# The padded halves of the attention state, summed from PSUM instead of copied from the state in SBUF

## The chip, the cores and the metric

The program runs on one core of a Trainium2 chip (trn2). The time is the device time of one execution in microseconds (us). Three runs of the kernel before gave 302.97, 303.89 and 305.05 us; the median is 303.89. Lower is better.

The core has five engines with a queue each: TensorE multiplies (its weight loads, PEld in the rows, run beside its matmuls, PE), VectorE (DVE) and ScalarE (ACT) work on SBUF and PSUM, GpSimd (POOL) on SBUF, and SyncE (SP) issues most of the transfers. An engine runs its queue in the order in which it is written; engines wait for one another by semaphores. PSUM has eight banks, and SBUF is the large memory on the chip.

## What is computed

Three parts follow one another. The first is a gated linear attention (batch 2, 8 heads, 768 tokens, head size 40). Per head it keeps a state C (40 x 40) and a vector n (40):

```
m_new  = max(f + m, i);  f_stab = exp(f + m - m_new);  i_stab = exp(i - m_new)
C = f_stab * C + i_stab * outer(v, k)
n = f_stab * n + i_stab * k
y = sigmoid(o) * (C @ q) / max(|n . q|, 1)
```

The second is an MLP over tokens and then one over channels, each with a residual and with a relu between its two products (768 -> 256 -> 768, 320 -> 1536 -> 320). The third is a gated projection: sigmoid of a causal convolution of five taps over x, times x @ w_val, the product times w_out. All is float32.

## The kernel before

The attention is done by chunks of 128 tokens: six per batch, twelve in all, numbered u. Within a chunk it is a masked product of q and k, weighted by exponentials of gate sums; between chunks the state is carried. A step is `attention(b, n)` with u = 6b + n, and n runs from 0 to 6: step n makes the masked product of chunk n, updates the state with chunk n and finishes y of chunk n - 1. All engines have a function of this name, and its order of lines is the order of the engine's queue.

The large products elsewhere are made more exact by splitting each float32 factor into a rounded part and a remainder (`_hi`, `_lo`): ScalarE makes hi of a weight (L671), GpSimd mostly lo (L539, L543), and TensorE runs three products for one. These splits of the later parts' weights (tok, ch, val, out) are laid among the attention's steps, by tables at the head of the program (`HI_AT`, `LO_POOL_AT`, `LO_VECTOR_AT`). Their staging buffers are shared: the load of a piece (`LOAD_AT`, issued by ScalarE at L397) waits until the piece before it in the same buffer has been split.

The steps of the first batch stand alone. After each of them from n = 4 on comes one chunk's share of the token MLP (`token_hidden`, L1252), which needs y_hi and y_lo of that chunk. The steps of the second batch are laid among the channel MLP of the first quarter of the tokens (L1177, L1315).

The state lies in SBUF as `state`, 104 partitions x 164: heads 0 to 3 in partitions 0 to 63, heads 4 to 7 in 64 to 103. The product that reads it (L1196) takes 128 rows, and it must see one group of heads at a time. So `apart` holds two padded copies, group 0 in one and group 1 in the other, with zeros elsewhere; there are two buffers of it, used in turn by even and odd chunks.

In step n of either batch VectorE runs in this order (n from 1 to 4; outside these some parts are missing):

1. multiplies the exponentials by q.k from PSUM, twice (`prob`, L958);
2. sums the new state: `delta` in PSUM, made by TensorE, plus `kept`, the decayed old state in SBUF (L969; in step 0 a copy, L966). This releases delta's PSUM bank;
3. finishes y of the chunk before: `den` (L978), the remainder `y_lo` of the chunk before that one (L948), `den` (L982), `rden` (L985), `yt` (L988);
4. makes the exponents of the next chunk, eight instructions (L939). ScalarE turns them into exponentials in place (L700);
5. copies the two halves of `state` into `apart` (L1003) and signals `apart_ready`.

GpSimd's step: `kept` (L583) from state and decay, `qs` = q times decay (L593), half of a weight's remainder (L539), `y` = yt times the output gate (L605, L606), which waits for yt, and `wv` (L572) for the next chunk. In the last step of the first batch VectorE makes this y itself (L1010, L1011). The last `token_hidden` of the first batch follows; ScalarE's `y_hi` for it stands behind ScalarE's split of a weight piece (L671) in that step.

PSUM's two banks `shared` serve all the small products (delta, y, hidden units and others) in turn; TensorE starts a product in one only when its last content was read (`begin`, L1166). In the second batch a step's delta, y and the hidden units before and behind them (`h_hi` L831 by ScalarE, `h_lo` L1107 by VectorE) share them.

## Time and profile before

| | before |
|---|---|
| median of three runs | 303.89 us |
| profiled execution | 303.86 us |
| its span, first to last instruction | 302.0 us |
| busy: TensorE matmul / weight load | 270.7 / 258.9 us |
| busy: VectorE | 203.2 us |
| busy: ScalarE / GpSimd | 122.6 / 88.0 us |
| transfers | 25.70 MB |

The profiled execution is 1.9 us longer than its span; what lies outside is start and end. In the page's 40 slices of 7.55 us each TensorE's matmuls are at 0.9 or more from 68 us on, up to the last three slices, and at 0.5 to 0.9 in most slices before. A busy time says how long an engine had an instruction under way: one that was under way but held up counts as busy.

### The profile page before, as it was taken

The page shows a single profiled execution, that of the slowest core. Times are in us where ns is not written, and L with a number is a line of the kernel's source. Part 1 is how long each engine was busy: PE and PEld are TensorE (multiplying, and loading weights), DVE is VectorE, ACT ScalarE, POOL GpSimd, SP SyncE. Part 2 cuts the span into 40 slices and gives each one's busy share as a digit, 9 for nine tenths or more (in the row PEclk, how much of TensorE's full clock was granted, in tenths as well). Part 3 has the DMA queues.
Part 4 walks back from the last instruction along what each step waited for, and adds up shares of the span by engine and source line. Part 5 has one row for each costly group of instructions (what it writes and reads, how often), then busy time and mean ns, then how long its engine had stood idle before and what let it go on. Part 6 is the DMA issues. An engine that isn't in the chain of part 4 may idle for free.

```text
span 302.0 us, 5376 instructions
## 1 busy us (share of the span) xinstructions
PE 270.7 (90%) x2024; PEld 258.9 (86%) x2024; DVE 203.2 (67%) x415; ACT 122.6 (41%) x225; POOL 88.0 (29%) x102
## 2 busy tenths in 40 slices
PE   0689678759999999999999999999999999999875
PEld 0577567659989999999899999999999999999774
DVE  7989999785698667866776521534674048762693
ACT  2656465226945453254333222432223333222623
POOL 4435755650066554324500400000012000040440
PEclk9959979796999999999999999999999999999979
DMA  7599964515567235322000001000000100000011
GB/s 219 159 305 306 294 178 123 174 30 208 173 161 243 77 90 150 88 80 67 0 0 3 0 22 46 0 2 0 0 3 0 64 4 0 2 0 1 24 43 65
DMA packets 26289, 25.70 MB, mean 85 GB/s; under 512 B 13976, under 2 KB 22008, under 8 KB 26264
## 3 DMA queue, kind: packets, MB, share of 16 engines
q1 hardware_dynamic: 21976, 18.72, 21.2%
q10 hardware_dynamic: 4288, 6.64, 6.8%
q8 instruction: 16, 0.26, 0.4%
q14 instruction: 9, 0.07, 0.1%
HBM read 23.34 MB, written 2.02 MB: 84 GB/s over the span
## 4 chain that ended last, share of the span: by engine, by line
PE 62%; DVE 10%; ACT 4%; issue 3%; DMA 2%; POOL 2%; ACTq 0%; DVEq 0%; POOLq 0%
PE shared L1177 25%; PE h_ps L1315 18%; DVE prob L939 3%; PE shared L1280 2%; PE s_ps L1215 2%; PE s_ps L1252 2%; PE shared L1265 2%; PE hv_ps L1196 2%; PE hv_ps L1200 1%; DMA stage<-val 1%; PE s_ps L1436 1%; DVE y_lo L948 1%; PE h_ps L1252 1%; PE shared L1284 1%; POOL x L628 1%
## 5 line engine op out<-in xcount | busy, mean ns | idle before, releaser
L1107 DVE SCALAR_TENSOR_TENSOR h_lo<-shared,h_hi 128x384 fp32r<-128x384 f32 x48 | 26.4, 557 | 35.0 <-ACT h_hi L831 34.8
L1315 PE MATMUL h_ps<-ch_hi,h_hi 128*128 128x320 f32 x144 | 45.4, 315 | 0.0
L831 ACT ACTIVATE h_hi<-shared 128x384 fp32r<-128x384 f32 x48 | 23.2, 489 | 53.5 <-PE shared L1177 50.7
L1315 PE MATMUL h_ps<-ch_hi,h_lo 128*128 128x320 f32 x144 | 44.5, 309 | 0.0
L1315 PE MATMUL h_ps<-ch_lo,h_hi 128*128 128x320 f32 x144 | 44.3, 308 | 0.0
L1177 PE MATMUL shared<-u_hi,ch_hi 128*128 128x384 f32 x96 | 32.9, 342 | 0.6 <-DVE yt L988 0.3
L1177 PE MATMUL shared<-u_lo,ch_hi 128*128 128x384 f32 x96 | 32.5, 339 | 0.0
L1177 PE MATMUL shared<-u_hi,ch_lo 128*128 128x384 f32 x96 | 32.5, 339 | 0.0
L1215 PE MATMUL s_ps<-q_in,k_in 128*128 128x128 f32 x192 | 27.5, 303 | 3.6 <-DMA q_in<-qT 3.5
L1215 PEld LDWEIGHTS s_ps<-q_in,k_in 128*128 128x128 f32 x192 | 25.6, 214 | 5.5 <-DMA q_in<-qT 4.2
L1043 DVE SCALAR_TENSOR_TENSOR gate<-x,conv_sb,gate 128x384 f32<-128x384 f32 x44 | 29.0, 667 | 1.0
L1315 PEld LDWEIGHTS h_ps<-ch_hi,h_hi 128*128 128x128 f32 x144 | 27.1, 188 | 0.4 <-DVE yt L988 0.2
L700 ACT ACTIVATE prob<-prob 128x512 f32<-128x512 f32 x24 | 14.9, 630 | 30.0 <-DVE prob L939 30.0
L1315 PEld LDWEIGHTS h_ps<-ch_lo,h_hi 128*128 128x128 f32 x144 | 27.1, 188 | 0.0
L1315 PEld LDWEIGHTS h_ps<-ch_hi,h_lo 128*128 128x128 f32 x144 | 27.0, 188 | 0.0
L1196 PE MATMUL hv_ps<-qs,apart 128*41 128x128 f32 x160 | 17.4, 298 | 7.0 <-DVE prob L958 6.4
L1200 PE MATMUL hv_ps<-prob,v_in 128*41 128x128 f32 x192 | 20.2, 304 | 1.2 <-DVE prob L958 1.2
L958 DVE TENSOR_TENSOR prob<-s_ps,prob 128x512 f32<-128x512 f32 x24 | 15.9, 687 | 7.7 <-PE s_ps L1215 7.5
L539 POOL TENSOR_TENSOR ch_lo<-stage,ch_hi 128x640 fp32r<-128x640 f32 (+1 forms) x8 | 13.3, 1680 | 21.7 <-ACT ch_hi L671 21.7
L1177 PEld LDWEIGHTS shared<-u_hi,ch_hi 128*128 128x128 f32 x96 | 18.0, 188 | 1.4 <-DVE yt L988 0.7
L605 POOL TENSOR_TENSOR y<-yt,o_sig 128x320 f32<-128x320 f32 x11 | 11.2, 1020 | 24.3 <-DVE yt L988 24.3
L1177 PEld LDWEIGHTS shared<-u_hi,ch_lo 128*128 128x128 f32 x96 | 18.0, 188 | 0.0
(191 smaller groups left out, 636.6 us busy)
## 6 DMA issues: line engine op xcount, KB each, us to landing
G_all<-G_scratch SPq DMA_DIRECT2D x11, 512.0 KB, 5.0
o_sig<-on ACTq DMA_DIRECT2D x2, 960.0 KB, 6.0
k_in<-kT SPq DMA_DIRECT2D x24, 80.0 KB
q_in<-qT SPq DMA_DIRECT2D x24, 80.0 KB
kn_in<-kn SPq DMA_DIRECT2D x12, 160.0 KB, 4.3
v_in<-vn SPq DMA_DIRECT2D x12, 160.0 KB, 4.8
stage<-ch ACTq DMA_DIRECT2D x3, 640.0 KB, 4.3
out<-o_sb SPq DMA_DIRECT2D x12, 160.0 KB, 1.8
```

The source lines that it names most:

```text
L539: eng.tensor_tensor(lo[:, half], raw[:, half], hi[:, half].bitcast(F32), ALU.subtract).then_inc(split[p], 1)
L605: pool.tensor_tensor(y32[:, 0:DM], yt[:], og, ALU.mult)
L700: act.activation(prob[w % 4][:], prob[w % 4][:], ACT.Exp).then_inc(exp_ready, 1)
L831: act.activation(h_hi[i % 3][:], ps_of(key)[:, 0:T], ACT.Relu).then_inc(hi_ready, 1)
L958: dve.tensor_tensor(prob[w % 4][:], s_ps[g][:], prob[w % 4][:], ALU.mult).then_inc(prob_ready, 1)
L1043: return dve.scalar_tensor_tensor(out=gate[:, d, :], in0=xt, scalar=w, in1=gate[:, d, :], op0=ALU.mult, op1=ALU.add)
L1107: took(dve.scalar_tensor_tensor(out=h_lo[i % 3][:], in0=ps_of(key)[:, 0:T], scalar=0.0, in1=h_hi[i % 3][:].bitcast(F32), op0=ALU.max, op1= ...
L1177: last = pe.matmul(out_ap, w, x, start=(n == 0), stop=(n == len(terms) - 1))
L1196: pe.matmul(hv_ps[64 * g:64 * g + D1, tile_cols(j)], apart[v % 2][:, g, j * D1:(j + 1) * D1], qs[v % 2][:, tile_cols(j)], start=True, stop ...
L1200: last = pe.matmul(hv_ps[64 * g:64 * g + D1, tile_cols(j)], v_in[v % 3][:, g * HG + j, :], prob[(2 * v + g) % 4][:, tile_cols(j)], start=( ...
L1215: last = pe.matmul(s_ps[g][:, tile_cols(j)], k_in[k_buffer(u)][:, g, tile_cols(j)], q_in[k][:, tile_cols(j)], start=True, stop=True)
L1315: last = pe.matmul(h2_ps[t][:, 0:DM], a[:, tile_cols(t)], w[:, f, :], start=(f == 0 and n == 0), stop=(f == FT - 1 and n == 2))
```

## The change

The two halves of `apart` are no longer copied from `state` at the step's end. They are summed (in step 0 copied) straight from delta's PSUM bank and `kept`, where the state is summed, each over its own partitions, and ahead of the state itself. `state` is still needed for the next `kept`, so its sum stays, but not in step 4, after which the batch needs no further state; there VectorE waits for its own last sum and releases the bank by an increment. The waits that guarded the copies move along: for the hidden matmuls that read this buffer of `apart` (`hv_ready`), and, at the start, for the zeroing of both buffers.

```diff
--- before.py
+++ after.py
@@ -959,14 +959,27 @@
                 if n < NC - 1:
                     key = ("delta", u)
                     full(dve, key)
-                    if u > 0:
-                        dve.wait_ge(apart_ready, with_next(u - 1))
-                    new, ps = state[:], ps_of(key)[0:ROWS, 0:HG * D1]
-                    if n == 0:
-                        took(dve.tensor_copy(new, ps), key)
+                    if u >= 1:
+                        dve.wait_ge(hv_ready, u)
+                    if n >= 1:
+                        dve.wait_ge(kept_ready, with_both(u))
+
+                    def grown(dst, r):
+
+                        ps = ps_of(key)[r, 0:HG * D1]
+                        if n == 0:
+                            return dve.tensor_copy(dst, ps)
+                        return dve.tensor_tensor(dst, ps, kept[r, :], ALU.add)
+
+                    new = apart[(u + 1) % 2]
+                    grown(new[0:64, 0, :], slice(0, 64))
+                    last = grown(new[64:ROWS, 1, :], slice(64, ROWS)).then_inc(apart_ready, 1)
+                    if n < NC - 2:
+                        last = grown(state[:], slice(0, ROWS))
+                        took(last, key)
                     else:
-                        dve.wait_ge(kept_ready, with_both(u))
-                        took(dve.tensor_tensor(new, ps, kept[:], ALU.add), key)
+                        dve.wait_ge(apart_ready, with_next(u))
+                        dve.sem_inc(shared_done[J[key] % 2], 1)
                 if (b, n) in LO_VECTOR_AT:
                     make_lo(dve, *LO_VECTOR_AT[b, n])
                 if n >= 1:
@@ -992,16 +1005,8 @@
                         ALU.mult), y_key)
                 if u == 0:
                     columns(1)
-                    dve.wait_ge(apart_zeroed, 2)
                 if n + 1 < NC:
                     exponents(u + 1)
-                if n < NC - 1:
-                    if u >= 1:
-                        dve.wait_ge(hv_ready, u)
-                    done(dve, key)
-                    for g, r in enumerate((slice(0, 64), slice(64, ROWS))):
-                        last = dve.tensor_copy(apart[(u + 1) % 2][r, g, :], state[r, :])
-                    last.then_inc(apart_ready, 1)
                 if (b, n) == (0, NC):
 
                     dve.wait_ge(o_ready, b + 1)
@@ -1073,6 +1078,7 @@
                     last.then_inc(a_lo_ready, 1)
 
             exponents(0)
+            dve.wait_ge(apart_zeroed, 2)
             for n in range(ATT_STEPS):
                 attention(0, n)
             exponents(NC, (0,))
```

VectorE's queue, first batch, from the end of step 3 (exponents of chunk 4) into step 4. `prob_`, `apart_` are buffers with their numbers; in brackets stands what an instruction waits for. Before:

```order
L939 SCALAR_TENSOR_TENSOR prob_109<-G_all_106,A_col,h_ps 128x128 x3
L1003 COPY apart_117<-state 64x164 [waits shared_done1,hv_ready]
L1003 COPY apart_117<-state 40x164
L958 TENSOR_TENSOR prob_108<-s_ps,prob_108 128x512 [waits s_ready,exp_ready]
L958 TENSOR_TENSOR prob_109<-s_ps,prob_109 128x512 [waits s_ready,exp_ready]
L969 TENSOR_TENSOR state<-shared,kept 104x164 [waits kept_ready,apart_ready,shared_full]
L978 TENSOR_SCALAR den<-shared 128x8 [waits shared_full]
L948 TENSOR_TENSOR y_lo<-y_121,y_hi 128x384 [waits split0,y_hi_ready]
L982 SCALAR_TENSOR_TENSOR den<-shared,den 128x8 [waits vector_step]
```

Now:

```order
L939 SCALAR_TENSOR_TENSOR prob_109<-G_all_106,A_col,h_ps 128x128 x3
L958 TENSOR_TENSOR prob_108<-s_ps,prob_108 128x512 [waits s_ready,exp_ready]
L958 TENSOR_TENSOR prob_109<-s_ps,prob_109 128x512 [waits s_ready,exp_ready]
L972 TENSOR_TENSOR apart_118<-shared,kept 64x164 [waits kept_ready,hv_ready,shared_full]
L972 TENSOR_TENSOR apart_118<-shared,kept 40x164
L991 TENSOR_SCALAR den<-shared 128x8 [waits apart_ready,shared_full]
L948 TENSOR_TENSOR y_lo<-y_121,y_hi 128x384 [waits split0,y_hi_ready]
L995 SCALAR_TENSOR_TENSOR den<-shared,den 128x8 [waits vector_step]
```

The copies between the exponents and the multiplications are gone; two sums follow the multiplications. This is step 4, in which the state's own sum is left out.

VectorE's queue, second batch, step 0, between the last multiplication and the hidden units `h_lo` of the channel MLP. Before:

```order
L966 COPY state<-shared 104x164 [waits apart_ready,shared_full]
L939 SCALAR_TENSOR_TENSOR prob_110<-G_all_107,A_col,mask_sb 128x128 [waits G_in1,hv_ready]
L939 SCALAR_TENSOR_TENSOR prob_110<-G_all_107,A_col,mask_sb 128x128 x3
L939 SCALAR_TENSOR_TENSOR prob_111<-G_all_107,A_col,mask_sb 128x128 [waits G_in1]
L939 SCALAR_TENSOR_TENSOR prob_111<-G_all_107,A_col,mask_sb 128x128 x3
L1003 COPY apart_118<-state 64x164 [waits shared_done0,hv_ready]
L1003 COPY apart_118<-state 40x164
L1107 SCALAR_TENSOR_TENSOR h_lo_87<-shared,h_hi_84 128x384 [waits hi_ready]
```

Now:

```order
L971 COPY apart_118<-shared 64x164 [waits hv_ready,shared_full]
L971 COPY apart_118<-shared 40x164
L971 COPY state<-shared 104x164
L939 SCALAR_TENSOR_TENSOR prob_110<-G_all_107,A_col,mask_sb 128x128 [waits G_in1,hv_ready]
L939 SCALAR_TENSOR_TENSOR prob_110<-G_all_107,A_col,mask_sb 128x128 x3
L939 SCALAR_TENSOR_TENSOR prob_111<-G_all_107,A_col,mask_sb 128x128 [waits G_in1]
L939 SCALAR_TENSOR_TENSOR prob_111<-G_all_107,A_col,mask_sb 128x128 x3
L1113 SCALAR_TENSOR_TENSOR h_lo_87<-shared,h_hi_84 128x384 [waits hi_ready]
```

The halves moved from behind the eight exponent instructions to a place ahead of them; they are copies from PSUM here, and the state's copy follows them.

## Rows read from the trace of the kernel before

**Rows 1.** Busy time by stretch, core 0.

```profile
15.00:67.00 52.00, 38.73 (x396) 34.69 (x396) 47.66 (x105) 25.12 (x39) 29.67 (x30) 0.86 0.69 201
67.00:82.00 15.00, 14.93 (x78) 14.19 (x79) 10.26 (x24) 11.29 (x16) 0.00 (x0) 0.79 0.55 180
82.00:140.00 58.00, 57.41 (x555) 53.84 (x554) 42.80 (x104) 26.09 (x47) 28.54 (x30) 1.00 0.45 131
```

**Rows 2.** The chain that ended last, first batch: start us, us, what.

```profile
52.48 0.73 DVE apart L1003
```

**Rows 3.** The removed copies in the second batch: ns min/median/max.

```profile
L1003 DVE COPY apart<-state x10: 226/238/244, 89.1 to 129.2; 64x164 f32<-64x164 f32 x5, 40x164 f32<-40x164 f32 x5
```

**Rows 4.** All copies together; then VectorE in time, steps 2 to 4.

```profile
L1003 DVE COPY apart<-state 64x164 f32<-64x164 f32 (+1 forms) x20 | 15.1, 757 | 0.1
...
34.37 3.97 DVE L1003 COPY apart<-state 64x164 f32<-64x164 f32 x2
...
43.25 3.72 DVE L1003 COPY apart<-state 64x164 f32<-64x164 f32 x2
...
51.89 2.36 DVE L1003 COPY apart<-state 64x164 f32<-64x164 f32 x2
```

**Rows 5.** GpSimd in time: start us, us, line, operation, idle before it.

```profile
29.33 1.80 POOL L539 TENSOR_TENSOR tok_lo<-stage,tok_hi 128x768 fp32r<-128x768 f32 x1
...
34.09 0.74 POOL L572 TENSOR_TENSOR wv<-v_in,w_col 128x328 f32<-128x328 f32 x1 [0.47 <-DMA v_in<-vn]
...
36.43 1.80 POOL L539 TENSOR_TENSOR tok_lo<-stage,tok_hi 128x768 fp32r<-128x768 f32 x1
41.35 0.87 POOL L605 TENSOR_TENSOR y<-yt,o_sig 128x320 f32<-128x320 f32 x1 [3.12 <-DVE yt L988]
...
44.80 1.82 POOL L539 TENSOR_TENSOR tok_lo<-stage,tok_hi 128x768 fp32r<-128x768 f32 x1
49.99 0.87 POOL L605 TENSOR_TENSOR y<-yt,o_sig 128x320 f32<-128x320 f32 x1 [3.37 <-DVE yt L988]
...
52.33 1.82 POOL L539 TENSOR_TENSOR tok_lo<-stage,tok_hi 128x768 fp32r<-128x768 f32 x1
...
61.94 3.85 POOL L539 TENSOR_TENSOR ch_lo<-stage,ch_hi 128x768 fp32r<-128x768 f32 x2 [1.62 <-ACT ch_hi L671]
```

**Rows 6.** VectorE instructions that read PSUM, by line and in time.

```profile
L969 DVE TENSOR_TENSOR state<-shared,kept x8: 319/319/330, 23.3 to 123.2; 104x164 f32<-104x164 f32 x8
...
L958 DVE TENSOR_TENSOR prob<-s_ps,prob x24: 680/691/693, 15.6 to 133.2; 128x512 f32<-128x512 f32 x24
...
29.05 0.32 DVE L969 TENSOR_TENSOR state<-shared,kept 104x164 f32<-104x164 f32 x1
```

**Rows 7.** Second batch, step 1: VectorE, TensorE, and TensorE's wait for h_lo.

```profile
92.36 0.32 DVE L969 TENSOR_TENSOR state<-shared,kept 104x164 f32<-104x164 f32 x1
...
93.28 0.34 PE L1177 MATMUL shared<-u_hi,ch_hi 128*128 128x384 f32 x1
...
PE shared L1226 <- DVE h_lo L1107: 0.6, 1, 0.6
```

**Rows 8.** VectorE instructions with two SBUF operands, first batch, in time.

```profile
29.35 2.20 DVE L948 TENSOR_TENSOR y_lo<-y,y_hi 128x384 fp32r<-128x384 f32 x1
...
39.88 0.55 DVE L948 TENSOR_TENSOR y_lo<-y,y_hi 128x384 fp32r<-128x384 f32 x1
...
62.26 1.87 DVE L1010 TENSOR_TENSOR y<-yt,o_sig 128x320 f32<-128x320 f32 x1
64.05 1.82 DVE L1011 TENSOR_TENSOR y<-yt,o_sig 128x64 f32<-128x64 f32 x1
```

**Rows 9.** The weight transfer (KB, us to landing) and ScalarE behind it.

```profile
stage<-ch ACTq DMA_DIRECT2D x1, 768.0 KB, 6.1
...
60.31 1.49 ACT L671 ACTIVATE ch_hi<-stage 128x1536 fp32r<-128x1536 f32 x1
```

**Rows 10.** TensorE's restart after the first batch, in time.

```profile
67.07 0.63 PE L1252 MATMUL h_ps<-y_hi,tok_hi 128*128 128x320 f32 x1 [3.40 <-DVE y_lo L948]
```

## The prediction

> **What bounds the kernel now.** I read the stretches first [rows 1]; the columns are the stretch, its length, the busy time of TensorE's matmuls, of its weight loads, of VectorE, ScalarE and GpSimd, then granted clock, DMA share and GB/s. While the second batch's attention runs between other matmuls (82 to 140 us) TensorE is busy 57.41 of 58.00 us, so only what makes it wait counts. In the first batch's attention (15 to 67 us) TensorE has 38.73 of 52.00 us and VectorE 47.66: this stretch is VectorE's. The chain of waits agrees: the second copy of step 4 stands in it [rows 2]. I call the step with index n "step n".
>
> Next, the 20 copies that the change removes. In the second batch the ten take 226 to 244 ns each, one after another [rows 3]. All 20 take 15.1 us, so the first batch's five pairs take 12.7, against 0.48 us a pair unhindered; those of steps 2, 3 and 4 take 3.97, 3.72 and 2.36 us [rows 4]. GpSimd explains it [rows 5]: in step 2 its wv starts at 34.09 and its queue runs without a gap to the end of tok_lo at 38.23; the copies start at 34.37 and end at 38.34. A copy from SBUF to SBUF waits for GpSimd here, and, with that queue back to back, for several of its instructions in a row.
>
> By the Trainium skill ("SBUF — State Buffer", Who interferes with whom) a float32 copy within SBUF may run in a two-port mode and then needs the port pair that GpSimd uses, while a VectorE instruction with at most one SBUF input outside these modes does not contend. Both halves agree with this trace: 3.97 us beside a busy GpSimd, and the next rows.
>
> What replaces the copies reads PSUM and at most one SBUF operand. All eight state sums take 319 to 330 ns and all 24 multiplications by s_ps 680 to 693 [rows 6]; the sum at 29.05 ran while GpSimd was about to pass from qs to tok_lo (29.33) and was not stretched. So I price a half at 0.32 us, not stretched.
>
> **The change part by part.**
> Two copies less per step, five steps per batch. First batch: on VectorE's path, and 12.7 us is the ceiling. Second batch: nothing comes back. The copies stood behind the eight exponent instructions, and what waits on those (the exponentials on ScalarE, then h_hi, then h_lo) had been released already.
>
> Two sums (or PSUM copies in step 0) more per step, now ahead of y and of the exponents. From the rows one sum takes 0.32 us whole; the next instruction behind the state sum at 92.36 overlapped its end, so two cost between 0.48 (the time of a copy pair) and 0.64 us [rows 3, 6]. I take the upper end, since no row shows halves overlapping. The skill ("VectorE: DVE Perf Modes", Two Vector instructions with no wait between them) says that an instruction whose output starts in another quadrant than the last one waits until that has finished; this speaks against the change. By it the ten steps would pay 6.4 us, without it 4.8.
>
> In step 4 of each batch the state sum goes (0.32 less), and a wait of VectorE for its own sums and an increment come in. No row prices it; between nothing and 0.32 us, a whole sum's time, it cancels at worst what goes.
>
> The buffer's bank is released after three reads, 0.64 us later. The tightest place is step 1 of the second batch: the state sum ran 92.36 to 92.68, and TensorE's next product started at 93.28 [rows 7]; 0.60 us of slack against 0.64. The wait for the hidden matmuls costs nothing: the same step's delta product stands behind them in TensorE's queue. The wait for the zeroed buffers, moved to the start, is long over.
>
> **What is late next.** Removing a stall only pays up to the next one, so I walk the first batch.
> Steps 0 and 1: the exponents of step 1 and what follows move by under 0.5 us either way; then y_lo at 29.35 took 2.20 us and ended at 31.55, 0.42 after GpSimd's tok_lo (29.33 to 31.13) [rows 5, 8]. y_lo has two SBUF operands and is held as the copies are. It ends then whether it comes early or not: no gain up to here, 34.37.
> Step 2: the exponents end at 34.37, and step 3 can begin. From the end of the copies (38.34) to y_lo (39.88) were 1.54 us; with 0.64 more y_lo is asked for at 36.6, or a microsecond later behind an exponential. GpSimd's tok_lo runs until 38.23, so y_lo ends at 38.65 where it ended at 40.43 (its 0.55 us began at 39.88) [rows 8]. Gain 1.78, not 3.97.
> From there GpSimd sets the pace: yt releases GpSimd's y, then come wv, kept, qs, tok_lo, then y_lo, den, rden, yt. From the start of y at 41.35 to the end of tok_lo at 46.62 are 5.27 us [rows 5]; 0.42 for y_lo's end and, from there to the next y, the 0.92 between 40.43 and 41.35 make 6.6, against 8.64 (y at 41.35 and 49.99). Gain 2.0 more. So y of step 4 starts near 46.2 in place of 49.99; from it to the end of tok_lo, 54.15, are 4.16 us as before, and that end comes near 50.4, 3.75 earlier.
> That tok_lo frees the buffer for the next weight transfer. It took 6.1 us and ScalarE's ch_hi started right behind it, at 60.31 [rows 9]. Now 50.4 + 6.1 = 56.5, ch_hi to 58.05, y_hi to 58.55. The last y_lo meets the first half of GpSimd's ch_lo (3.85 us for two, 1.9 each, from 58.05), ends at about 60.3, and TensorE starts the last token_hidden. It started at 67.07 [rows 10]. Gain 6.7: 3.75 from the transfer, 2.95 because VectorE's two y products, 1.87 and 1.82 us beside ch_lo at 62 to 66 [rows 8], now run before ch_lo does.
> If y_lo waits for both halves of ch_lo, 1.9 us go: gain 4.8. If the transfer is faster by a microsecond, gain 7.7.
> Behind 67 the chain is TensorE, ScalarE and loads in the same order, and moves with it.
>
> Second batch: in step 0 the 0.64 us stand ahead of the exponents, whose exponentials hold up h_hi and h_lo, and TensorE waited 0.6 us for h_lo already [rows 7]. I charge 0.6 here and nothing elsewhere, between 0 (the exponents were held by GpSimd's ch_lo anyway) and 1.0.
>
> **The sum.** 303.86 (profiled execution; the median of three is 303.89) - 6.7 + 0.6 = 297.8. The forecast's own range is a gain of 4.8 - 1.0 to 7.7 + 0.3: 295.8 to 300.1.
>
> **Rivals.**
> 1. *The loads pace it.* If the weight transfer at 50.4 lands 3 us later, since everything ahead of it on the queues is now packed closer, ch_hi and the last y_lo are 3 us later: gain 3.7 - 0.6, 300.8. For it: DMA share 0.69 in the stretch [rows 1], and 6.1 us for the transfer. Against: the transfer of G ahead of it moves by about as much. Chance 0.13.
> 2. *More than computed.* TensorE pauses for less before the last token_hidden than the 3.40 us of [rows 10], and keeps its clock. From 67 to 82 us it was granted 0.79 of it [rows 1]; with only the two levels of 2.4 and 1.2 GHz that is 6.3 us of 15 at the lower one, and at the upper these would take 3.1 less. Two thirds of it: 295.7. Against: ScalarE and the loads share this path. Chance 0.08.
> 3. *Slower: the second batch pays and the first gives nothing.* Place: the shared bank at [rows 7], in every step with 0.6 us of slack or less. Price 0.64 us in five steps, 3.2 in all; with y_lo and tok_lo taking the whole of the first batch's stall, 307.1. It decides if the sums halt TensorE in each step; most have more slack, and 3.97 and 3.72 us of stall have nothing to fill them. Chance 0.05.
> 4. *No change.* The halves read from PSUM are held by GpSimd as the copies were, because kept lies in SBUF: then VectorE stands as before, 303.9 to 304.9. 32 unstretched instructions speak against [rows 6], though few of the state sums lay beside a busy GpSimd. Chance 0.09.
> The forecast keeps 0.65.
>
> **Numbers.** A change of 1% (3.0 us) is about what can be told here. Faster by more (below 300.9): forecast, rival 2 and most of rival 1, 0.84. Within: 0.11. Slower: 0.05. Forecast and rival 1 hold 0.78, so the range goes from 295.3, into rival 2, to 300.9.
>
> **What would show it.** The half sums at 0.32 us beside a busy GpSimd; y_lo in steps 3, 4 and 5 stretched to 1.3 us and more and ending 0.4 us after tok_lo; GpSimd's y of step 4 near 46.2; the last token_hidden near 60.3; the two y products near 0.4 us. In the second batch about 1.2 us of waiting for h_lo in place of 0.6. It is wrong if the half sums are stretched, if TensorE restarts within 2 us of 67, or if its waits after 82 grow beyond 1.5 us.

## The result, and the profile after

Four runs of the changed kernel gave 298.65, 299.74, 300.29 and 300.83 us, median 300.01; four of the kernel before gave a median of 304.39. The ratio is 0.985 with a 95% interval of 0.982 to 0.989: 1.5% faster. The ratios in this document leave out runs that took over 1.5% longer than the fastest of their kernel, two of four in experiment 5 and two of ten in experiment 7. The forecast was 297.8 (295.3 to 300.9), faster with 0.84. The profiled execution took 298.65 us with a span of 296.9, against 303.86 and 302.0: 5.1 us less in the spans; it is the fastest of the four.

These are the stretches of the changed kernel, with the columns of [rows 1]; the cuts lie where the same work begins, 7 to 8 us earlier than there.

```profile
15.00:60.00 45.00, 36.42 (x412) 32.72 (x411) 38.84 (x106) 25.53 (x39) 27.81 (x30) 0.92 0.83 244
60.00:75.00 15.00, 14.72 (x86) 13.72 (x87) 10.37 (x25) 12.05 (x17) 2.09 (x2) 0.89 0.53 175
75.00:144.00 69.00, 65.83 (x602) 61.22 (x600) 54.57 (x116) 28.37 (x54) 34.67 (x37) 1.00 0.37 105
```

The first batch is 7 us shorter and VectorE's busy time in it falls from 47.66 to 38.84. The third line is the second batch up to the first `x` that follows it; the same stretch before the change is

```profile
83.00:149.00 66.00, 65.08 (x600) 61.08 (x599) 48.80 (x117) 28.95 (x54) 34.66 (x37) 1.00 0.38 110
```

So the first batch gave more than was forecast, and the second took some of it back: 3 us more for the same work, with TensorE idle for 3.17 us of it where it was idle for 0.92.

VectorE's groups by line answer [rows 4, 6]: busy us and mean ns of one. L972 and L971 are the new half sums and half copies (20 in all, 16 + 4), L939 with mask_sb the exponents of the second batch, L1015 and L1016 the last y products of [rows 8].

```profile
L939 DVE SCALAR_TENSOR_TENSOR prob<-G_all,A_col,mask_sb 128x128 f32<-128x128 f32 x40 | 21.4, 603 | 0.0
L948 DVE TENSOR_TENSOR y_lo<-y,y_hi 128x384 fp32r<-128x384 f32 x12 | 15.1, 1261 | 2.4 <-ACT y_hi L707 2.2
L972 DVE TENSOR_TENSOR apart<-shared,kept 64x164 f32<-64x164 f32 (+1 forms) x16 | 5.2, 322 | 0.1
L971 DVE COPY apart<-shared 64x164 f32<-64x164 f32 (+1 forms) x4 | 1.3, 320 | 0.0
L1015 DVE TENSOR_TENSOR y<-yt,o_sig 128x320 f32<-128x320 f32 x1 | 0.5, 493 | 0.1
L1016 DVE TENSOR_TENSOR y<-yt,o_sig 128x64 f32<-128x64 f32 x1 | 0.2, 219 | 0.0
```

15.1 us of copies became 6.5 us of half sums. The exponents were 17.3 us before (mean 500 ns) and `y_lo` 11.1 (925 ns): what the copies no longer wait for, two other kinds of instruction wait for in part.

VectorE and then GpSimd in time, from steps 3 to 5 of the first batch, and the last `y_lo` (compare [rows 4, 5, 8]):

```profile
36.17 0.66 DVE L972 TENSOR_TENSOR apart<-shared,kept 64x164 f32<-64x164 f32 x2
37.17 1.74 DVE L948 TENSOR_TENSOR y_lo<-y,y_hi 128x384 fp32r<-128x384 f32 x1
...
44.12 1.40 DVE L948 TENSOR_TENSOR y_lo<-y,y_hi 128x384 fp32r<-128x384 f32 x1
...
58.17 1.92 DVE L948 TENSOR_TENSOR y_lo<-y,y_hi 128x384 fp32r<-128x384 f32 x1 [0.91 <-ACT y_hi L707]
```

```profile
36.67 1.82 POOL L539 TENSOR_TENSOR tok_lo<-stage,tok_hi 128x768 fp32r<-128x768 f32 x1
39.83 0.87 POOL L605 TENSOR_TENSOR y<-yt,o_sig 128x320 f32<-128x320 f32 x1 [1.34 <-DVE yt L1001]
...
46.44 0.86 POOL L605 TENSOR_TENSOR y<-yt,o_sig 128x320 f32<-128x320 f32 x1 [1.33 <-DVE yt L1001]
...
48.77 1.81 POOL L539 TENSOR_TENSOR tok_lo<-stage,tok_hi 128x768 fp32r<-128x768 f32 x1
```

The half sums at 36.17 lie within GpSimd's `qs` and the start of `tok_lo` (its queue is busy from 34.32 to 38.49) and still take 0.33 us each; `y_lo` behind them is held and ends at 38.91, 0.42 after `tok_lo`. The last `tok_lo` ends at 50.58, the weight transfer issued at 50.61 lands after 5.6 us, and ScalarE and TensorE follow (answering [rows 9] and [rows 10]):

```profile
56.24 1.49 ACT L671 ACTIVATE ch_hi<-stage 128x1536 fp32r<-128x1536 f32 x1 [1.17 <-DMA stage<-ch]
```

```profile
60.15 0.41 PE L1258 MATMUL h_ps<-y_hi,tok_hi 128*128 128x320 f32 x1 [2.66 <-DVE y_lo L948]
```

The second batch, step 2, in time: VectorE, then GpSimd.

```profile
94.36 0.67 DVE L972 TENSOR_TENSOR apart<-shared,kept 64x164 f32<-64x164 f32 x2
95.06 0.33 DVE L972 TENSOR_TENSOR state<-shared,kept 104x164 f32<-104x164 f32 x1
95.37 1.91 DVE L948 TENSOR_TENSOR y_lo<-y,y_hi 128x384 fp32r<-128x384 f32 x1
98.04 6.28 DVE L939 SCALAR_TENSOR_TENSOR prob<-G_all,A_col,mask_sb 128x128 f32<-128x128 f32 x8
```

```profile
95.29 1.58 POOL L539 TENSOR_TENSOR ch_lo<-stage,ch_hi 128x640 fp32r<-128x640 f32 x1 [3.20 <-ACT ch_hi L671]
98.20 0.92 POOL L605 TENSOR_TENSOR y<-yt,o_sig 128x320 f32<-128x320 f32 x1 [1.33 <-DVE yt L1001]
...
100.18 0.80 POOL L572 TENSOR_TENSOR wv<-v_in,w_col 128x328 f32<-128x328 f32 x1 [0.74 <-DMA v_in<-vn]
100.94 0.51 POOL L583 TENSOR_TENSOR kept<-state,decay 104x164 f32<-104x164 f32 x1
101.41 1.26 POOL L593 TENSOR_TENSOR qs<-q_in,decay 128x512 f32<-128x512 f32 x1
102.64 1.53 POOL L539 TENSOR_TENSOR ch_lo<-stage,ch_hi 128x640 fp32r<-128x640 f32 x1
```

Before, the same step read, on VectorE and on GpSimd:

```profile
102.77 0.55 DVE L948 TENSOR_TENSOR y_lo<-y,y_hi 128x384 fp32r<-128x384 f32 x1
...
104.07 3.36 DVE L939 SCALAR_TENSOR_TENSOR prob<-G_all,A_col,mask_sb 128x128 f32<-128x128 f32 x8
```

```profile
103.11 1.63 POOL L539 TENSOR_TENSOR ch_lo<-stage,ch_hi 128x640 fp32r<-128x640 f32 x1 [3.10 <-ACT ch_hi L671]
...
107.78 0.74 POOL L572 TENSOR_TENSOR wv<-v_in,w_col 128x328 f32<-128x328 f32 x1 [1.82 <-DMA v_in<-vn]
```

`y_lo` used to start 0.34 us ahead of `ch_lo`; now it starts 0.08 behind it and takes 1.36 us more. The exponents therefore start late, and GpSimd's next chain (`wv`, `kept`, `qs`, `ch_lo`), which used to start after their end, now runs through them: 6.28 us in place of 3.36, ending with that chain. TensorE's waits after 74 us show what it costs (us in total, times, longest), where there were 0.6 for `h_lo` [rows 7] and 0.3 for `yt`, and the row in time shows the longer of the two at the `delta` product of the step behind:

```profile
PE shared L1232 <- DVE h_lo L1113: 2.3, 2, 1.9
PE shared L1183 <- DVE yt L1001: 0.9, 1, 0.9
```

```profile
106.01 0.76 PE L1232 MATMUL shared<-wv,kn_in 128*64 128x41 f32 x16 [1.85 <-DVE h_lo L1113]
```

### The profile page after: what moved, and what is told of

Same layout as the page of the kernel before. It is cut to its first block, busy times and chain, and to the rows that moved or that the text cites. A ratio compares the mean times of both kernels' runs of the same rounds, so it can differ in the third digit from the quotient of the medians.

```text
span 296.9 us, 5367 instructions
## 1 busy us (share of the span) xinstructions
PE 265.7 (90%) x2024; PEld 253.4 (85%) x2024; DVE 199.4 (67%) x413; ACT 121.7 (41%) x225; POOL 88.0 (30%) x102
## 4 chain that ended last, share of the span: by engine, by line
PE 53%; DVE 22%; ACT 7%; issue 4%; DMA 4%; POOL 3%; ACTq 0%; DVEq 0%; POOLq 0%
PE shared L1183 24%; PE h_ps L1321 16%; DVE prob L939 9%; DVE y_lo L948 4%; DVE gate L1048 2%; PE s_ps L1221 2%; DMA stage<-ch 2%; PE shared L1286 2%; PE s_ps L1258 2%; DVE apart L972 1%; ACT prob L700 1%; PE shared L1271 1%; DVE prob L958 1%; DMA stage<-val 1%; POOL x L628 1%
## 5 line engine op out<-in xcount | busy, mean ns | idle before, releaser
L939 DVE SCALAR_TENSOR_TENSOR prob<-G_all,A_col,mask_sb 128x128 f32<-128x128 f32 x40 | 21.4, 603 | 0.0
L1206 PE MATMUL hv_ps<-prob,v_in 128*41 128x128 f32 x192 | 18.7, 285 | 1.4 <-DVE prob L958 1.4
```

The lines of the kernel that those rows point to most:

```text
L939: last = dve.scalar_tensor_tensor(out=prob[(2 * u + g) % 4][:, tile_cols(j)], in0=G_all[u % 2][:, tile_cols(h)], scalar=A_col[:, col:col + ...
L1206: last = pe.matmul(hv_ps[64 * g:64 * g + D1, tile_cols(j)], v_in[v % 3][:, g * HG + j, :], prob[(2 * v + g) % 4][:, tile_cols(j)], start=( ...
```

## The experiments

Two theories stood at the start. **A**: the first batch gains as walked, and the second loses because VectorE comes later there and its instructions with two SBUF inputs now overlap GpSimd's. **B** and **C** in the expectations are the rivals each of them names. In what follows two lengths are read from each profile: from the start to the first `h_lo` of the channel MLP (the first batch and what hangs on it), and from there to the first `x` behind the second batch. What comes after is the same in all 13 profiles: 152.9 to 153.1 us to the end of the span. With them goes what happens in step 2 of the second batch:

```
                               first  h_lo    y_lo starts, us       wv starts behind   exponents
kernel                         h_lo   to x    (ch_lo starts)        the exponents      take
before                         83.03  65.96   102.77 0.55 (103.11)  3.71               3.36
changed                        74.96  68.96    95.37 1.91  (95.29)  2.14               6.28
changed, once more             75.73  69.14    96.12 1.90  (96.04)  1.87               6.28
first batch only               75.57  66.82    96.32 0.55  (96.66)  3.28               3.36
first batch only, once more    76.78  66.10    96.73 0.55  (97.08)  4.80               3.36
second batch only              83.78  66.65   104.19 0.55 (104.15)  3.84               3.34
place alone, both batches      77.46  69.58    98.31 1.77  (98.09)  1.93               6.28
place alone, first batch       77.32  65.86    97.06 0.55  (97.40)  4.24               3.36
source alone, first batch      75.94  65.94    95.65 0.55  (95.99)  3.37               3.36
first batch, delay in second   74.51  68.24    95.08 0.55  (95.02)  2.09               6.78
first batch, tok_lo behind y   79.80  65.84    99.52 0.55  (99.87)  4.53               3.35
changed, ch2_lo later          74.46  66.56    94.83 0.55  (none)   3.09               2.87
first batch, ch2_lo later      74.86  65.89    94.59 0.55  (none)   3.28               2.87
```

**1. The change in the first batch only.**

```diff
+                    if b == 0:
+                        ... (the sums of the halves, as in the change)
+                    else:
+                        ... (the state's sum, as before)
...
+                if n < NC - 1 and not (b == 0):
+                    ... (the copies behind the exponents, as before)
...
```

> The change in the first batch's steps alone; the second batch copies the halves from state behind the exponents as before. Theory A: in the changed kernel the first batch gained some 8 us by the time the second batch's attention begins, and 3 us were lost in the second batch, because the two sums ahead of y move VectorE's instructions with two SBUF operands (y_lo, exponents) 0.65 us later, into GpSimd's ch_lo, kept and qs. Then this kernel is about 3 us faster than the changed one, near 297 us; the 40 exponents of the second batch are back near 17 us (21.4 in the changed kernel) and TensorE's waits between the start of the second batch's attention and the third part stay below 1.5 us (3.5 in the changed kernel). Theory B: the loss comes from the first batch's being earlier, which shifts loads and ScalarE's ch_hi against GpSimd and VectorE; then the time stays near 300 and the exponents near 21 us.

Measured: median 296.38 us (295.17 to 299.35, six runs) against 304.15, ratio 0.974 (0.969 to 0.979): faster than the changed kernel. The exponents take 18.0 us, and TensorE restarts at

```profile
59.65 0.64 PE L1275 MATMUL h_ps<-y_hi,tok_hi 128*128 128x320 f32 x1 [3.54 <-DVE y_lo L948]
```

and never waits for `h_lo`. The whole gain is the first batch's. The weight transfer behind the last `tok_lo` takes 4.5 us here, and `ch_hi` starts at 53.71, 2.5 us ahead of the changed kernel's; TensorE's restart comes only 0.5 us sooner. GpSimd's `ch_lo`, from 55.34 on, now catches the second y product, and the last `y_lo` starts late:

```profile
55.67 1.83 DVE L1033 TENSOR_TENSOR y<-yt,o_sig 128x64 f32<-128x64 f32 x1
58.09 1.50 DVE L948 TENSOR_TENSOR y_lo<-y,y_hi 128x384 fp32r<-128x384 f32 x1 [0.59 <-ACT y_hi L707]
```

**2. The change in the second batch only.** The same edit with `b == 1`.

> The change in the second batch's steps alone. Theory A: nothing is won and the second batch loses, by 0.6 us where no new meeting with GpSimd comes about and by up to 3 where it does: 305 to 307.4 us. Theory B: as before, 304.4, within 0.5.

Measured: 306.16 us (303.76 to 307.63, ten runs), ratio 1.005 (1.001 to 1.010). The first batch's ten copies take 15.4 us (12.7 before). The profile shows 0.69 us more than before in the second stretch, but no stretched exponents: `wv` comes 3.84 us behind their start, too late to meet them.

```profile
104.19 0.55 DVE L948 TENSOR_TENSOR y_lo<-y,y_hi 128x384 fp32r<-128x384 f32 x1
...
105.49 3.34 DVE L939 SCALAR_TENSOR_TENSOR prob<-G_all,A_col,mask_sb 128x128 f32<-128x128 f32 x8
```

So in this profile moving the sums ahead costs 0.7 us by itself. The other 2.3 of the changed kernel need the meeting in step 2, and this kernel misses the first part of it by little: its `y_lo` starts 0.04 us behind `ch_lo` and isn't held. The profiled run (305.18) is among the shorter of the ten; the median lies 2.0 us above that of the kernel before, and what the longer runs met was not profiled.

**3. The place alone.** The halves are copied from `state` in SBUF as before, but right behind its sum, in both batches.

```diff
                         took(dve.tensor_tensor(new, ps, kept[:], ALU.add), key)
+                    if u >= 1:
+                        dve.wait_ge(hv_ready, u)
+                    done(dve, key)
+                    for g, r in enumerate((slice(0, 64), slice(64, ROWS))):
+                        last = dve.tensor_copy(apart[(u + 1) % 2][r, g, :], state[r, :])
+                    last.then_inc(apart_ready, 1)
... (the same lines behind the exponents go)
```

> The halves are still copied from state in SBUF, but right behind the state's sum, where the changed kernel sums them from PSUM (VectorE waits for its own sum first). It tells place from source. Theory A1 (source: only what reads PSUM escapes GpSimd): the copies are held by GpSimd in the first batch at the new place as well, and the time stays near 304. Theory A2 (place): at the new place the copies are held by qs and tok_lo, but y_lo right behind them was to be held until the end of the same tok_lo anyway, so the copies cost only some 0.3 us each, and the first batch gains nearly as much as in the changed kernel: 300 to 302 us, with the copies' busy time still well above 10 us.

Measured: 299.24 us (297.51 to 301.76), ratio 0.983 (0.977 to 0.990), as good as the changed kernel though the copies still read SBUF. VectorE in time, first batch, steps 3 and 4:

```profile
36.59 1.91 DVE L974 COPY apart<-state 64x164 f32<-64x164 f32 x2
38.72 0.56 DVE L948 TENSOR_TENSOR y_lo<-y,y_hi 128x384 fp32r<-128x384 f32 x1
43.91 1.91 DVE L974 COPY apart<-state 64x164 f32<-64x164 f32 x2
46.05 0.56 DVE L948 TENSOR_TENSOR y_lo<-y,y_hi 128x384 fp32r<-128x384 f32 x1
```

The copies are held to the end of the same `tok_lo` that would have held `y_lo`, which then runs free: one hold in place of the other. In the second batch this kernel meets GpSimd as the changed one does.

**4. The source alone.** First batch: the halves are summed from PSUM, but at the old place, behind the exponents, the bank released there. Second batch as before.

```diff
... (in the first batch the state's sum no longer releases the bank)
+                    if b == 0:
+                        half = ps_of(key)
+                        for g, r in enumerate((slice(0, 64), slice(64, ROWS))):
+                            dst, src = apart[(u + 1) % 2][r, g, :], half[r, 0:HG * D1]
...
+                                last = dve.tensor_tensor(dst, src, kept[r, :], ALU.add)
+                        last.then_inc(apart_ready, 1)
+                        dve.wait_ge(apart_ready, with_next(u))
+                        dve.sem_inc(shared_done[J[key] % 2], 1)
...
```

> The other half of the pair: in the first batch the halves are summed from PSUM and kept, but at the old place behind the exponents (the bank is released there); the second batch is as before. If the source alone is enough, the ten instructions take 0.32 us each and none is held, the first batch gains about 7 us until TensorE's restart, and the time is 296.5 to 298. If the place is what pays, 304. A later release of delta's bank could cost up to 1 us, since TensorE's next delta product waits for it.

Measured: 297.50 us (296.57 to 298.80), ratio 0.977 (0.972 to 0.983); the sums take

```profile
L1011 DVE TENSOR_TENSOR apart<-shared,kept 64x164 f32<-64x164 f32 (+1 forms) x8 | 2.6, 322 | 0.1
```

and TensorE restarts at 60.91. In the first batch the source alone brings most of the gain: 6.7 us of the medians, where experiment 1 beside it has 7.8, and the intervals of the two overlap. Experiment 10 tries the place alone there.

**5. The changed kernel once more.** No edit.

> The changed kernel as it is, beside the next three on one chip, and a second profile of it. If the second batch's loss comes from a meeting of VectorE's y_lo and exponents with GpSimd's queue, the second profile shows exponents stretched by microseconds at one or two of its steps again (sum of the 40 at 20 us or more, 17.3 before) and the time is 299 to 301 us.

Measured: median 299.45 us of four runs (295.07 to 299.91). Three of them lie at 299.2 to 299.9, and the ratio (0.976, 0.967 to 0.984) says little. The profile, of the run of 299.74, repeats the pattern:

```profile
96.12 1.90 DVE L948 TENSOR_TENSOR y_lo<-y,y_hi 128x384 fp32r<-128x384 f32 x1
98.78 6.28 DVE L939 SCALAR_TENSOR_TENSOR prob<-G_all,A_col,mask_sb 128x128 f32<-128x128 f32 x8
```

TensorE restarts as early as in the first profile of this kernel (60.15):

```profile
60.07 0.64 PE L1258 MATMUL h_ps<-y_hi,tok_hi 128*128 128x320 f32 x1 [2.74 <-DVE y_lo L948]
```

One run of 295.07 us stands apart. No profile of such a run exists; that in it `y_lo` was not held, as in experiment 2, is possible and not shown.

**6. The changed kernel, with GpSimd's remainder of the third piece of ch2 one step later.**

```diff
-              (1, 0): (6, 0), (1, 1): (6, 1), (1, 2): (7, 0), (1, 3): (7, 1),
+              (1, 0): (6, 0), (1, 1): (6, 1), (1, 3): (7, 0), (1, 4): (7, 1),
```

> The changed kernel, with GpSimd's splits of the last third of ch2 moved from steps 2 and 3 of the second batch to steps 3 and 4. Theory A (y_lo of step 2 met the ch_lo that starts as it does, so the exponents behind it met wv, kept, qs and the next ch_lo): y_lo of step 2 takes 0.55 us and not 1.9, the exponents of step 2 about 3 us and not 6.3, and up to 3 us come back, 297 to 298.5. Against it: the moved ch_lo meets the exponents or y_lo one step later, or TensorE waits for the third piece; then 299.5 or more.

Measured: 296.98 us (295.90 to 297.50), ratio 0.975 (0.971 to 0.978). VectorE, step 2, and the group of exponents:

```profile
94.83 0.55 DVE L948 TENSOR_TENSOR y_lo<-y,y_hi 128x384 fp32r<-128x384 f32 x1
96.14 2.87 DVE L939 SCALAR_TENSOR_TENSOR prob<-G_all,A_col,mask_sb 128x128 f32<-128x128 f32 x8
```

```profile
L939 DVE SCALAR_TENSOR_TENSOR prob<-G_all,A_col,mask_sb 128x128 f32<-128x128 f32 x40 | 16.0, 468 | 0.0
```

With `ch_lo` gone from step 2 the stretch falls from 68.96 to 66.56 us: 2.4 of the 3.0 us come back, and 0.6 stays, the price of the sums' place. This bears out theory A for the second batch.

**7. First batch only, with GpSimd's remainder of tok behind its y.** If `y_lo` waits for `tok_lo`, let it come first.

```diff
-                if (b, n) in LO_POOL_AT:
+                if b == 1 and (b, n) in LO_POOL_AT:
                     make_lo(pool, *LO_POOL_AT[b, n])
...
                                        ALU.mult).then_inc(y32_ready, 1)
+                if b == 0 and (b, n) in LO_POOL_AT:
+                    make_lo(pool, *LO_POOL_AT[b, n])
```

> As the kernel with the change in the first batch alone, and in the first batch GpSimd's weight split stands behind its y, not ahead of it. It asks whether y_lo held by tok_lo is what paces the first batch now. If so, y_lo takes 0.55 us in steps 2 to 4, but GpSimd's own round (y, split, wv, kept, qs) is as long as it was, 5.3 us plus 1.3, so each step is shortened by at most 0.5 us and the time is 295.5 to 297.5. If wv, kept and qs, which now stand behind the split, come late for TensorE, up to 2 us slower.

Measured: 303.42 us (ten runs, 300.55 to 307.00), ratio 0.997 (0.993 to 1.001): the gain is gone and the expectation missed. `y_lo` is free in steps 2 to 5 (0.55 to 0.63 us), but the split ends later, and the split is what others wait for:

```profile
PE h_ps L1277 <- POOL tok_lo L539: 2.5, 1, 2.5
```

```profile
55.91 1.80 POOL L539 TENSOR_TENSOR tok_lo<-stage,tok_hi 128x768 fp32r<-128x768 f32 x1
...
63.42 3.92 POOL L539 TENSOR_TENSOR ch_lo<-stage,ch_hi 128x768 fp32r<-128x768 f32 x2 [5.02 <-ACT ch_hi L673]
```

The last `tok_lo` ends at 57.71, where the two profiles of experiment 1's kernel have 49.20 and 50.39; the transfer starts behind it, and TensorE restarts at 65.70 in place of 59.65 and 60.86. That the end of the last `tok_lo` paces the end of the first batch is what the prediction rested on; here it is shown by delaying it. Whether the delay came by the transfer or by TensorE's own wait for `tok_lo` (the first row), this run doesn't separate.

**8. First batch only, with the delay of the second put in.** In the second batch half sums are made ahead of the state's sum and the copies stay, so VectorE is later by the sums and nothing else changes.

```diff
...
+                        for g, r in enumerate((slice(0, 64), slice(64, ROWS))):
+                            dst, src = apart[(u + 1) % 2][r, g, :], ps_of(key)[r, 0:HG * D1]
...
+                                dve.tensor_tensor(dst, src, kept[r, :], ALU.add)
...
```

> The kernel with the change in the first batch alone, and in the second batch the two half sums from PSUM are made as well, ahead of the state's sum, while the copies behind the exponents stay (the halves are written twice). Theory A: the 0.65 us ahead of y and the exponents is all that costs, so 3 us are lost again, near 299.5 us, with the exponents at 20 us or more. Theory C: the loss came with taking the copies away from behind the exponents (they kept VectorE off GpSimd's queue or the other way round); then it stays near 296.5.

Measured: 297.69 us (296.90 to 298.17), ratio 0.977 (0.974 to 0.980). The delay alone stretches the exponents to 21.9 us and makes TensorE wait 1.8 us for `h_lo`; the stretch is 68.24 us, 1.4 to 2.1 above the two profiles of the first batch only. The median is 1.3 us above that of experiment 1, which ran on another chip, and the intervals of the two ratios overlap; near 299.5 was expected. So it is the profile, and not the median, that shows the loss. Here `y_lo` started 0.06 us behind `ch_lo` and was not held; in the changed kernel it started 0.08 behind and was held; the exponents were caught all the same, since `wv`, which waits for `v_in`, started early, 2.09 us behind their start.

**9. The best of both.** First batch only, with the edit of experiment 6.

> The change in the first batch alone, as in the first experiment, and with it GpSimd's two halves of the remainder of the third piece of the second channel weight (ch2_lo) a step later (in steps 3 and 4 of the second batch, where they were in steps 2 and 3). Theory A (the first batch gives its 8 us whatever the second does; the second costs by what GpSimd and VectorE do at the same time in its step 2): nothing is stretched there any more, the 40 exponents take 16 to 17 us in all (18.0 in the first experiment, 21.4 in the changed kernel), TensorE starts the last token_hidden at 59.5 to 60.5, and the time is 295.5 to 296.5 us, 0.5 to 1 below the first experiment beside it. Rival (the exponents of the first experiment's second batch are held but behind nothing that TensorE waits for): the exponents are as short, and the time is that of the first experiment within 0.3 us. Rival B (what the faster first batch gives is lost again to the loads of the second batch): no gain, and waits for stage or weights in the stretch behind 75 us.

Measured: 296.44 us (295.48 to 298.20, six runs), ratio 0.975 (0.971 to 0.978). The exponents take 16.7 us and the second stretch 65.89, as before the change; but experiment 11 beside it has the same median. Once the exponents aren't caught, what is left of their stretching is hidden: the rival holds.

**10. The place alone, first batch only.** The edit of experiment 3 under `if b == 0`, the second batch as before.

> First batch alone again, but only the place is changed: the halves are still copied from state in SBUF, right behind the state's sum, ahead of y. The second batch is as before the change. Theory A2 (in the first batch the place suffices: the copies are held by GpSimd until tok_lo ends, but y_lo behind them would have been held by the same tok_lo, so one hold takes the place of the other): copies of steps 2 to 4 of about 1.9 us a pair, y_lo behind them 0.56 us, last token_hidden between 59.7 and 61.5, time 296.3 to 298.3, at most 1.5 us above the first experiment beside it. Rival (source alone: without the sums from PSUM the stall only moves): last token_hidden not before 64 and time above 300.

Measured: 298.25 us (295.82 to 299.52, six runs), ratio 0.980 (0.976 to 0.984), 1.8 us above experiment 11 where at most 1.5 was expected; TensorE restarts at 62.38, outside the expected 59.7 to 61.5. So the place alone brings some three quarters of the gain (6.1 us of the medians against 7.9). The rest is this:

```profile
37.31 1.91 DVE L975 COPY apart<-state 64x164 f32<-64x164 f32 x2
39.46 0.56 DVE L948 TENSOR_TENSOR y_lo<-y,y_hi 128x384 fp32r<-128x384 f32 x1
```

`y_lo` ends at 40.02, 1.14 us behind `tok_lo` (37.06 to 38.88), where in the changed kernel it ends 0.42 behind; GpSimd's period from one `tok_lo` to the next is 7.33 us (37.06 to 44.39) against 6.61 (36.67 to 43.28). With PSUM as source, what follows the sums already waits inside the hold.

**11. Experiment 1 once more, beside 9 and 10.** No edit.

> The first experiment (the change in the first batch alone) once more, beside the two others, so that they have something to be compared with on the same chip. Expected 296.4 us as before, between 295.5 and 297.5, a ratio to the kernel before of 0.970 to 0.980; last token_hidden at 59.5 to 60; exponents 18 us in all. If it is above 298 the spread between chips is as large as what the other two are to tell apart, and they decide nothing.

Measured: 296.45 us (294.39 to 298.57, six runs), ratio 0.974 (0.969 to 0.979), within 0.1 us of experiment 1. Its profiled run restarts at 60.86, a microsecond later than expected.

## Why the prediction was right, and where it was off

- **The copies waited for GpSimd, and the half sums don't**: 0.31 to 0.33 us each as priced (0.32), 20 of 20. A pair takes 0.65 to 0.67 us, the upper of the two ends. The rule of the Trainium skill that speaks against the change ("VectorE: DVE Perf Modes", Two Vector instructions with no wait between them) fits: the second half starts in another quadrant of partitions and doesn't overlap the first. The sum of 6.4 us by it compares with 6.5 measured.
- **y_lo is late next**: in steps 3 and 4 of the first batch it ended at 38.91 (38.65 forecast) and 45.52, each 0.42 to 0.43 behind `tok_lo`. GpSimd's period was 6.61 us against 6.6 forecast (39.83 to 46.44), y of step 4 came at 46.44 (46.2). In step 5 it took 0.61 us, where the prediction had wanted 1.3 or more: it started only 0.19 us ahead of the end of `tok_lo`, and ended 0.42 behind it; nothing hung on that.
- **The transfer and the restart**: `tok_lo` ended at 50.58 (50.4), `ch_hi` started at 56.24 (56.5), the y products took 0.49 and 0.22 us (about 0.4 wanted), TensorE restarted at 60.15 (60.3). The gain there is 6.92 us against 6.7. Experiment 7 shows that the end of `tok_lo` carries it. The branch "If the transfer is faster by a microsecond, gain 7.7" is wrong: in the two profiles of the first batch only it took 4.5 and 4.7 us, yet TensorE restarted 10.45 and 10.47 us behind the end of `tok_lo`, later than the changed kernel's 9.57. An earlier `ch_lo` catches the second y product (1.83 and 1.84 us in place of 0.22), and the last `y_lo` then ends 0.4 us behind the second half of `ch_lo`, not the first.
- **Rival 2, more than computed**, came true in part: from the restart to the first `h_lo` passed 14.81 us where it had been 15.96 (67.07 to 83.03), with 0.88 of the clock granted in that stretch against 0.80. TensorE had paused 2.66 us before its restart in place of 3.40. That gave 1.15 us in this run. The other profile of the changed kernel (experiment 5) paused 2.74 us and yet took 15.66, at a clock of 0.82: there it gave 0.30. Over all 13 profiles the stretch follows the granted clock, which at 1.00 is the upper of its two levels (2.4 GHz) throughout and below that a mix with the lower (1.2 GHz): 15.8 to 16.0 us at 0.80 and 0.81, 15.4 at 0.85, 14.8 to 15.1 at 0.88 and 0.89, 14.1 at 1.00 (experiment 7). The pause alone doesn't tell which it will be: 2.79 us in experiment 8 went with 0.89, 2.74 in experiment 5 with 0.82, and 3.54 with 0.81 in experiment 1 and 0.85 in experiment 3.
- **The second batch: the term that was mis-sized.** The step said: "I charge 0.6 here and nothing elsewhere, between 0 (the exponents were held by GpSimd's ch_lo anyway) and 1.0." It measured 3.0 us (68.96 against 65.96), 3.2 in the second profile. The 0.6 is there (0.69 in experiment 2, 0.60 in experiment 6, both without the meeting); the other 2.4 is a meeting with GpSimd in step 2, which no step of the prediction looked for. The hold of `y_lo` there starts the exponents 1.35 us late (11.79 us behind those of step 1, 10.44 before), and their stretching starts those of step 3 later by 1.26 more (11.79 against 10.53). The prediction walked the first batch instruction by instruction against GpSimd and charged the second by one wait. The text also named its own alarm, waits after 82 beyond 1.5 us: TensorE's waits for `h_lo` and `yt` are 3.2 where they were 0.9. By that sign the account of the second batch was wrong, though the total fell within the range.
- **Rivals 1, 3 and 4** did not come: the transfer took 5.6 us, not 9; the first batch gave all it had; the sums weren't held.

The sum then is 303.86 - 6.9 - 1.15 + 3.0 = 298.8, and the profiled execution took 298.65. Without the meeting it would have been 2.4 less (an estimate from experiment 6).

**Luck** is in it too. The forecast gain was 6.1 us, and the medians moved by 4.4; 300.01 lies 2.2 above the forecast and 0.9 inside the upper bound. That bound was set for a late transfer (rival 1), which did not come; the second batch used up the room. In the profiled run the clock gave back 1.15 us of that loss, in the other profile 0.30.

**Faster than both** is the change in the first batch only: 296.4 us in twelve runs on two chips, 3 to 3.6 below the changed kernel's medians, with a ratio (0.974, at most 0.979) clear of the changed kernel's 0.982 to 0.989. The changed kernel with `ch_lo` a step later (experiment 6, 297.0) comes close to it.

## What to carry to other kernels

Two engines that exclude each other on SBUF make a stall wherever their instructions meet, so an instruction moved by 0.6 us is priced by what it will run beside: write down, for the steps behind it too, which instruction of the other engine starts first. Apply such a change only where its stall is, since elsewhere it can bring only the delay. And of two engines that wait for one another, ask whose end others wait for before giving the other one the lead.

## What the runs showed of the hardware

- Who is held turns on less than 0.1 us. In step 2 of the second batch `y_lo` started 0.08 us behind `ch_lo` and took 1.9 us (in both profiles of the changed kernel); started 0.04 and 0.06 behind it (experiments 2 and 8), it took 0.55, and `ch_lo` took 2.01 and 2.04 in place of 1.58. GpSimd's times in a profile are rough, so the boundary itself isn't measured. The Trainium skill ("SBUF — State Buffer", Who interferes with whom) says that the port pair shared by VectorE and GpSimd is an exclusive lock, and that the order of issue decides which of the two is blocked; both outcomes occur here.
- The exponents (two SBUF inputs and a scalar per partition) are caught by chains: in step 2 of the second batch eight took 2.87 us free, 6.28 to 6.78 where GpSimd's `wv` started 1.87 to 2.14 us behind their start, and 3.36 or less where it started 3.09 or more behind. In step 3, in the kernels that had this meeting, `wv` started 1.4 us behind their start, no `ch_lo` stood behind `qs`, and they took 4.8. In step 2 `wv` starts when `v_in` has landed, which varied by 2.1 us against the first `h_lo` among these kernels (23.97 in experiment 8, 26.05 in experiment 11).
- A held instruction can wait for several GpSimd instructions in a row: the copies 3.7 to 4.0 us a pair [rows 4], and `y_lo` too. In experiment 4 it started within `qs` (27.49 to 28.76) and ended at 30.95, 0.42 behind the `tok_lo` that followed `qs` without a gap (to 30.53); the same came again at 43.93.

```profile
28.58 2.37 DVE L948 TENSOR_TENSOR y_lo<-y,y_hi 128x384 fp32r<-128x384 f32 x1
```

It isn't always so: of the pair at 34.37 [rows 4] the first copy started within `wv` and took 0.55 us, and the second then took 3.40, through `kept`, `qs` and `tok_lo`. What decides whether an instruction is let in between two of GpSimd's was not settled.
